# Expert tiles: the second layer in two halves with the next tile's transposes between them, activation copies ahead of weight splits, the last tile in its own PSUM bank

## The reference, cut to what matters

```
attention (decayed linear attention, B=4, H=8, S=768, D=64)  -> x [3072, 512]
x = softplus(x @ w_in [512, 2048]) @ w_out [2048, 512]        dense layer
logits = x @ w_gate [512, 8];  expert_idx = argmax(logits);  gate_w = its softmax value
for e in range(8):                                            routed layer
    xe  = x[expert_idx == e]
    out[expert_idx == e] = gate_w * (relu(xe @ w1[e] [512, 1024]) @ w2[e] [1024, 512])
```

## Time and profile before

| | |
|---|---|
| median of three executions | 1017.44 us |
| the profiled execution | 1015.7 us, its span 1013.9 us |
| TensorE matmuls busy | 985.8 us (97% of the span) |
| VectorE / ScalarE / GpSimd busy | 494.6 / 436.2 / 155.8 us |
| second layer, L1470, 696 matmuls | 167.1 us busy, 6.7 us idle before them |
| first layer, L1445, 696 matmuls | 172.1 us busy, 0.0 us idle before them |
| share of the chain that ended last | PE 89%, DVE 4%, "issue" 3% |

### The profile page before, as it was taken

One profiled execution on the slowest core, in us unless ns is written; L12 is line 12 of the kernel. 1 busy time (PEld: TensorE's weight loads), 2 busy tenths in 40 slices (PEclk: granted clock), 3 DMA queues, 4 the chain that ended last, 5 costly groups with the idle time before them and its releaser, 6 DMA issues.

```text
span 1013.9 us, 17631 instructions
## 1 busy us (share of the span) xinstructions
PE 985.8 (97%) x5968; PEld 854.2 (84%) x5969; DVE 494.6 (49%) x1003; ACT 436.2 (43%) x756; POOL 155.8 (15%) x171
## 2 busy tenths in 40 slices
PE   6999999999999999999999999999999999999995
PEld 5888888888888888888888988888888888888873
DVE  3654464454455455455456696563223423335553
ACT  2764444444444444543544556233223323335541
POOL 3012101001002002001000002022122222233330
PEclk9999999999999999999999999999999999999997
DMA  8523211211111112112111014165111211452830
GB/s 329 188 100 129 74 40 45 65 33 62 59 38 61 45 35 78 42 38 79 30 44 43 32 47 148 48 220 194 50 44 36 112 60 43 187 210 64 334 129 11
DMA packets 28774, 91.83 MB, mean 91 GB/s; under 512 B 4062, under 2 KB 4190, under 8 KB 23584
## 3 DMA queue, kind: packets, MB, share of 16 engines
q1 hardware_dynamic: 23904, 76.48, 21.4%
q0 software_dynamic: 4800, 14.42, 4.4%
HBM read 78.30 MB, written 13.89 MB: 91 GB/s over the span
## 4 chain that ended last, share of the span: by engine, by line
PE 89%; DVE 4%; issue 3%; ACT 1%; DMA 1%; DVEq 1%; ACTq 0%; POOL 0%; SPq 0%; POOLq 0%
PE ps L1356 25%; PE ps L1339 25%; PE ps L1470 15%; PE ps L1445 14%; PE ps L1252 3%; PE ps L1260 2%; PE ps L1455 2%; PE ps L1277 1%; PE ps L1429 1%; PE ps L1269 1%; DVE arena L858 1%; DMA arena<-table 1%; DMA arena<-x_rows,arena 1%; ACT W L692 0%; DVEq L1189 0%
## 5 line engine op out<-in xcount | busy, mean ns | idle before, releaser
L1356 PE MATMUL ps<-W,GS 128*128 128x512 f32 x1152 | 280.0, 396 | 1.8 <-DVE GS L847 1.8
L1339 PE MATMUL ps<-XS,W 128*128 128x384 f32 x1536 | 278.9, 336 | 2.1 <-DVE XS L810 1.6
L1339 PEld LDWEIGHTS ps<-XS,W 128*128 128x128 f32 x1536 | 269.4, 188 | 8.0 <-DVE XS L810 1.8
L1356 PEld LDWEIGHTS ps<-W,GS 128*128 128x128 f32 x1152 | 212.3, 188 | 51.1 <-issue 3.1
L1470 PE MATMUL ps<-W,XS 128*128 (+1 forms) x696 | 167.1, 396 | 6.7 <-DVE XS L1083 6.7
L1445 PE MATMUL ps<-W,XS 128*128 (+1 forms) x696 | 172.1, 396 | 0.0
L843 DVE SCALAR_TENSOR_TENSOR arena<-ps,arena 128x384 f32<-128x384 f32 x128 | 71.3, 557 | 204.7 <-ACT arena L642 204.5
L1470 PEld LDWEIGHTS ps<-W,XS 128*128 128x128 f32 x696 | 129.6, 190 | 34.1 <-issue 8.4
L638 ACT ACTIVATE arena<-ps 128x384 f32<-128x384 f32 x128 | 62.8, 491 | 221.4 <-PE ps L1339 188.8
L1445 PEld LDWEIGHTS ps<-W,XS 128*128 128x128 f32 x696 | 129.6, 190 | 25.8
L858 DVE CUSTOM_DVE_ANT_0 arena<-arena 128x512 bf16<-128x512 f32 x168 | 117.4, 738 | 0.0
(11 more groups left out here) (167 smaller groups left out, 611.0 us busy)
## 6 DMA issues: line engine op xcount, KB each, us to landing
arena<-w SPq DMA_DIRECT2D x32, 1024.0 KB, 6.8
arena<-kT SPq DMA_DIRECT2D x24, 256.0 KB, 2.7
arena<-qT SPq DMA_DIRECT2D x24, 256.0 KB, 3.2
arena<-v SPq DMA_DIRECT2D x24, 256.0 KB, 4.1
arena<-k SPq DMA_DIRECT2D x24, 256.0 KB, 4.3
x_rows<-arena SPq DMA_DIRECT2D x24, 256.0 KB, 4.7
arena<-w_out SPq DMA_DIRECT2D x4, 1024.0 KB, 5.1
arena<-w_in SPq DMA_DIRECT2D x3, 1024.0 KB, 5.1
```

What stands on the lines that cost most here:

```text
L1339: last = pe.matmul(ps_h[g % 2], w_in_s[a][:, g // 4, k_, (g % 4) * P:(g % 4 + 1) * P], xs[half][b][:, k_, :], start=(k_ == 0 and a + b == ...
L1356: last = pe.matmul(ps_x[s], GS[:, g % 2, a, s * P:(s + 1) * P], w_out_s[b][:, g, :], start=(g == 0 and a + b == 0), stop=(g == GF - 1 and ...
```

## The change

- TensorE's tile j becomes: second half of `mm2(j-1)`, `mm1(j+1, 0)`, `mm1(j+1, 1)`, first half of `mm2(j)`, `h_transpose(j+1)`, `x_transpose(j+2)`. `mm2` takes the half n as an argument and counts `s_m2` twice a tile.
- ScalarE's tile j becomes: two `relu(j+1)`, `h_high(j+1, 0)`, `tile_x_high(j+2)`, `h_high(j+1, 1)`, then `refill(j+1, 0)` and `refill(j, 1)`. VectorE's becomes `h_low(j+1, 0)`, `tile_x_low(j+2)`, `scale_y(j)`, `h_low(j+1, 1)`, `refill(j+1, 0)`, `refill(j, 1)`. w2 is thus refilled one iteration after w1 of the same visit, where it was two.
- The slot is computed as `visit & 1` in registers instead of read from a table.
- The last tile's second layer goes to bank 6 and does not wait for bank 5.
- Tiles 4 to 22 are written out on TensorE (no loop). The other engines keep their loops.
- The wait for the last scatter moves from GpSimd to SP.

```diff
@@ -243,7 +243,7 @@
 
         ps_h1 = [ps[:, 3, :], ps[:, 4, :]]
         ps_th = [ps[:, 1, :], ps[:, 2, :]]
-        ps_tx, ps_y2 = ps[:, 0, :], ps[:, 5, :]
+        ps_tx, ps_y2, ps_y_last = ps[:, 0, :], ps[:, 5, :], ps[:, 6, :]
 
         ps_rank0, ps_inv0 = ps[:, 2, 0:(EC + 1) * E], ps[:, 1, 0:5 * TA]
         ps_xT = [ps[:, 5 + i, :] for i in range(SUB)]
@@ -465,6 +465,7 @@
                 load_weights(r, 0)
                 load_weights(r - 1, 1)
             load_weights(E - 1, 1)
+            sp.wait_ge(s_end, 16)
 
 
         @block.gpsimd
@@ -578,7 +579,6 @@
                                     ).then_inc(s_end, 16)
             for q in range(2):
                 pool.wait_ge(s_sc[q], n_sc[q])
-            pool.wait_ge(s_end, 16)
 
 
         @block.scalar
@@ -703,12 +703,11 @@
                     act.wait_ge(s_th, 2 * t)
                 act.activation(h_sb[:, n * 512:(n + 1) * 512], ps_h1[n], ACT.Relu).then_inc(s_relu, 1)
 
-            def h_high(t):
-                for n in range(2):
-                    act.wait_ge(s_th, 2 * t + n + 1)
-                    if not (isinstance(t, int) and t == 0):
-                        act.wait_ge(s_m2, t)
-                    act.activation(th[0][:, n * 512:(n + 1) * 512], ps_th[n], ACT.Copy).then_inc(s_thi, 1)
+            def h_high(t, n):
+                act.wait_ge(s_th, 2 * t + n + 1)
+                if not (isinstance(t, int) and t == 0):
+                    act.wait_ge(s_m2, 2 * t + n - 1)
+                act.activation(th[0][:, n * 512:(n + 1) * 512], ps_th[n], ACT.Copy).then_inc(s_thi, 1)
 
             tile_x_high(0)
             copy_out(NBLK - 1)
@@ -720,13 +719,16 @@
             relu(0, 1)
             tile_x_high(1)
             exp_of(late_wide[0], 2)
-            h_high(0)
+            h_high(0, 0)
+            h_high(0, 1)
             relu(1, 0)
             relu(1, 1)
             tile_x_high(2)
             act.wait_ge(s_sel, 1)
             act.activation(slots.rearrange("p (c w t) -> p c w t", w=2, t=TT)[:, :, 0, :],
                            sel.rearrange("p (c t) -> p c t", t=TT), ACT.Copy, scale=tok).then_inc(s_sl, 1)
+            h_high(1, 0)
+            h_high(1, 1)
 
             def steer(j):
 
@@ -736,25 +738,24 @@
 
                 with act.If(flag > 0):
                     visit = act.value_load(visit_i[0:1, at1(j)], min_val=0, max_val=E - 1)
-                    par = act.value_load(parity_i[0:1, at1(j)], min_val=0, max_val=1)
                     if which:
-                        act.wait_ge(s_m2, j + 1)
+                        act.wait_ge(s_m2, 2 * j + 2)
                     else:
                         act.wait_ge(s_m1, 2 * j + 2)
-                    split_high(visit + 2, bass.ds(par, 1), which)
+                    split_high(visit + 2, bass.ds(visit & 1, 1), which)
 
             def tile(j, ahead=2, refills=True):
-                if refills and ahead >= 1:
-                    before, after = steer(j - 1), steer(j + 1)
-                h_high(j)
-                if ahead >= 1:
-                    relu(j + 1, 0)
-                    relu(j + 1, 1)
+                if refills:
+                    here, after = steer(j), steer(j + 1)
+                relu(j + 1, 0)
+                relu(j + 1, 1)
+                h_high(j + 1, 0)
                 if ahead >= 2:
                     tile_x_high(j + 2)
-                if refills and ahead >= 1:
-                    refill(j - 1, 1, before)
+                h_high(j + 1, 1)
+                if refills:
                     refill(j + 1, 0, after)
+                    refill(j, 1, here)
 
             for j in range(1, TA):
                 tile(j, refills=False)
@@ -765,7 +766,6 @@
             with act.Fori(TA, NT0 - 1) as j:
                 tile(j)
             n_tiles = act.value_load(ntile_i[0:1, 0:1], min_val=NT0, max_val=NT)
-            final = act.value_load(ntile_i[0:1, 1:2], min_val=NT0 - 1, max_val=NT - 1)
             def ending(j):
 
                 with act.If(n_tiles > j):
@@ -775,7 +775,6 @@
                         act.sem_inc(s_left, 1)
 
             ending(NT0)
-            h_high(final)
 
 
         @block.vector
@@ -1076,15 +1075,14 @@
                 dve.wait_ge(s_uhi, t + 1)
                 dve.tensor_tensor(tx[1], ps_tx, tx[0].bitcast(F32), ALU.subtract).then_inc(s_ulo, 1)
 
-            def h_low(t):
-                for n in range(2):
-                    dve.wait_ge(s_thi, 2 * t + n + 1)
-                    cols = slice(n * 512, (n + 1) * 512)
-                    dve.tensor_tensor(th[1][:, cols], ps_th[n], th[0][:, cols].bitcast(F32),
-                                      ALU.subtract).then_inc(s_tlo, 1)
+            def h_low(t, n):
+                dve.wait_ge(s_thi, 2 * t + n + 1)
+                cols = slice(n * 512, (n + 1) * 512)
+                dve.tensor_tensor(th[1][:, cols], ps_th[n], th[0][:, cols].bitcast(F32),
+                                  ALU.subtract).then_inc(s_tlo, 1)
 
             def scale_y(t, q, sc):
-                dve.wait_ge(s_m2, t + 1)
+                dve.wait_ge(s_m2, 2 * t + 2)
                 if sc is not None:
                     dve.wait_ge(s_sc[q], sc)
                 dve.tensor_scalar(y_sb[q], ps_y2, gate_s[:, at1(t)], None, ALU.mult).then_inc(s_y, 1)
@@ -1167,22 +1165,27 @@
             dve.wait_ge(s_lg, 1)
             done(dve.tensor_copy(logits[:, NCH - SUB:NCH, :], by(ps_lg, E)))
             choose(EC, NCH, late, late_wide)
-            h_low(0)
+            h_low(0, 0)
+            h_low(0, 1)
             gate_parts(EC, NCH, late[2], late_wide[0], 2)
             route_tiles()
             tile_x_low(2)
+            h_low(1, 0)
             scale_y(0, 0, None)
+            h_low(1, 1)
             late_indices()
-            h_low(1)
             steering()
+            h_low(2, 0)
             tile_x_low(3)
             scale_y(1, 1, None)
+            h_low(2, 1)
             slot_gates()
-            h_low(2)
+            late_gates()
+            h_low(3, 0)
             tile_x_low(4)
-            late_gates()
+            scale_y(2, 0, 16)
+            h_low(3, 1)
             split_low(1, 1, 0)
-            scale_y(2, 0, 16)
 
             def steer(j):
 
@@ -1191,28 +1194,25 @@
             def refill(j, which, flag):
                 with dve.If(flag > 0):
                     visit = dve.value_load(visit_i[0:1, at1(j)], min_val=0, max_val=E - 1)
-                    par = dve.value_load(parity_i[0:1, at1(j)], min_val=0, max_val=1)
-                    split_low(visit + 2, bass.ds(par, 1), which)
+                    split_low(visit + 2, bass.ds(visit & 1, 1), which)
 
             def tile(j, q, sc, ahead=2):
-                if ahead >= 1:
-                    before, after = steer(j - 1), steer(j + 1)
-                h_low(j)
+                here, after = steer(j), steer(j + 1)
+                h_low(j + 1, 0)
                 if ahead >= 2:
                     tile_x_low(j + 2)
-                if ahead >= 1:
-                    refill(j - 1, 1, before)
                 scale_y(j, q, sc)
-                if ahead >= 1:
-                    refill(j + 1, 0, after)
-
-            h_low(TA - 1)
+                h_low(j + 1, 1)
+                refill(j + 1, 0, after)
+                refill(j, 1, here)
+
+            h_low(TA, 0)
             tile_x_low(TA + 1)
+            scale_y(TA - 1, 1, 16)
+            h_low(TA, 1)
             split_low(1, 1, 1)
             dve.wait_ge(s_tabs, 1)
-            flag = steer(TA)
-            scale_y(TA - 1, 1, 16)
-            refill(TA, 0, flag)
+            refill(TA, 0, steer(TA))
             with dve.Fori(TA // 2, NT0 // 2 - 1) as i:
                 tile(2 * i, 0, 16 * i)
                 tile(2 * i + 1, 1, 16 * i)
@@ -1228,9 +1228,8 @@
                         dve.sem_inc(s_left, 1)
 
             ending(NT0)
-            h_low(final)
-            dve.wait_ge(s_m2, final + 1)
-            dve.tensor_scalar(y_last, ps_y2, gate_s[:, at1(final)], None, ALU.mult).then_inc(s_y, 1)
+            dve.wait_ge(s_m2, 2 * final + 2)
+            dve.tensor_scalar(y_last, ps_y_last, gate_s[:, at1(final)], None, ALU.mult).then_inc(s_y, 1)
 
 
         @block.tensor
@@ -1446,28 +1445,28 @@
                                          start=(k_ == 0 and a + b == 0), stop=(k_ == KD - 1 and a == 1))
                 last.then_inc(s_m1, 1)
 
-            def h_transpose(t, last=False):
+            def h_transpose(t):
                 for n in range(2):
                     pe.wait_ge(s_relu, 2 * t + n + 1)
                     if not (isinstance(t, int) and t == 0):
-                        pe.wait_ge(s_tlo, 2 * t if last else 2 * t + n - 1)
+                        pe.wait_ge(s_tlo, 2 * t + n - 1)
                     for k_ in range(4):
                         last = pe.transpose(ps_th[n][:, k_ * P:(k_ + 1) * P],
                                             h_sb[:, (4 * n + k_) * P:(4 * n + k_ + 1) * P], eye)
```

(77 more changed lines are left out.)

## The result

The changed kernel is slower. Six executions have a median of 1023.87 us (1021.72 to 1031.42) where the kernel before has 1015.91 in the same comparison; the ratio of the means is 1.0094, with a 95% interval of 1.0054 to 1.0135. A second measurement of the same kernel gave 1.0096 (1.0062 to 1.0131, median 1027.34). The forecast was 7.1 us faster.

What follows compares the result with a forecast made beforehand. TensorE's chain of 12.24 us a tile was taken as the bound, winnable only where TensorE stood still; 5.5 + 4.6 - 4.4 + 1.4 = 7.1 us less than the median 1017.4 gives 1010.3, range 1005.0 to 1016.0.

Steps and rivals of the forecast that it cites:

- Part 1: TensorE's second layer waiting for VectorE's low part of h: transposes between the halves remove all 5.5 us of stalls.
- The slack of 1.0 us of the x part: Tightest step of the new order: x part usable at 14.0 us after a tile's start, due for `mm1` at 15.0.
- Part 3: ScalarE's split of late w2 delays `relu` and h transposes in tiles 17, 20, 23, 24: costs 4.4 us, bounds 2.2 and 8.2.
- I take 12.5, between the two, and 10.7 for the third: Assumed us from a burst's first issue on SP to landing of its fourth load (12.5) and third load (10.7).
- the bound of 13.6: Latest landing of a burst's loads, 13.6 us after first issue, when traffic falls off; gives 1.9 us for tiles 17 and 20.
- Part 2: Last tile on TensorE: the 3.5 us lost and 1.4 of low clock go, less 0.28 of issue, a gain of 4.6 us.
- part 4: TensorE's tiles written out, slot from the visit number: extra sequencer work covered by the engine's queue, 0 us.
- (c): Rival outside the forecast's range, counted with anything else that makes the kernel slower; chance 0.08.
- Part 5: End of kernel, last scatter's wait on SP: GpSimd's drain begins right after the issue, the end comes 1.4 us sooner.
- (a): Rival: w2 is never late, 11.5 us less, 1005.9; chance 0.25.
- (b): Rival: the stalls are moved, all bounds against the change and no drain gain, 1.9 us less, 1015.5; chance 0.20.
- The signs to look for: Trace signs, among them w2 splits waiting for DMA in tiles 17 and 20, over 2 us idle around tile 24.

Runs made afterwards that it cites:

- the first experiment: Changed kernel with one edit in SP's queue, w2 of visit r-1 loaded ahead of w1 of visit r: 1009.88 us, ratio to before 0.9937.

## Why the prediction was wrong, point by point

**Part 1, the stalls of VectorE's low part: right.** All 5.5 us went, and a tile without a refill is 12.23 us as computed. The slack of 1.0 us of the x part held: no first layer of the changed kernel waits for it, and with the loads in the new order one does, by 0.42 us, behind the four split pieces.

**Part 3, the late w2: right mechanism, mis-sized, and this decides.** The place, the chain and the tiles were as forecast, as the idle times and the first experiment show. The step that failed is "I take 12.5, between the two, and 10.7 for the third": from the first issue ScalarE could go on after 15.5 and 13.2 us in the first burst, 17.2 and 14.2 in the second. The first issue came at 861.48, 8.69 us after the tile's start at 852.79, where 8.7 was forecast; it is the landing alone. Put into the forecast's own chain, 15.5 and 17.2 give waits of 4.0 and 5.7 us; 3.4 and 5.2 were measured from end to start.

Two readings misled. The largest time to landing, 7.7, does not fit the last load of a burst: issued 3.8 us after the first, it would have landed at 11.5, and the traffic lasted to 13.6. In the changed kernel's profile the same row gives 13.3. And the bound of 13.6 was one burst's; in the burst that begins at 858.47 in the same trace the queues are still full (430 GB/s) at 872. The spacing was short as well: the third and fourth load were issued 0.5 us apart and landed 2.3 and 3.0 us apart, where 1.8 had been taken. The stalls of tiles 17 and 20 became 3.3 and 5.0 us, not 0.1 to 1.9; the one of tile 24 became 3.4, where 2.4 was forecast for tiles 23 and 24 together, and 0 to 1 more for tile 24's own w2.

**A term was missing: the price of the clock behind a new stall.** The prediction charged 1.4 us of it to the old kernel's last tile and nothing to the stalls it forecast itself, which at 1.0 us each would hardly have cost any: behind 1.74 us of idle time in the kernel before, 24 matmuls took 5.75 us, where 5.71 is usual. At 3 to 5 us they cost 8.2 us more between tiles 10 and 27. With 12.9 idle instead of 4.4, and these 8.2, the term is 21.2 where 4.4 stood. That is the slowest of the six executions; how the 7.5 us that separate it from the median divide into idle time and clock, no trace shows. The Trainium skill, "TensorE: Matmul & The Clock Gate", section on oscillation in real kernels, has this as its pattern: idle gaps that let the clock fall, so that the work after each is paid at the low rate. The trace agrees: 4.43 us for twelve matmuls, in a stretch at a mean clock of 0.60, behind a gap of 3.27 us.

**Part 2, the last tile: the copies' cover was right, the gain did not come.** The 2.76 us wait for VectorE is gone and 3.13 us of issue are in its place, with the low clock behind it as before. The step that failed is in part 4, "it has half of its time free" and the 0 that is drawn from it: it looked at addresses and register loads and not at the branch of the ending, 3.5 us in the trace of before, which had 4.2 us of work over it. The change left 2.8 us there, and the branch itself came out at 4.6 us. Its sentence that "the trace shows no such stall here" is true of the loop alone; at the ending the same trace has a branch of 3.5 us that only the engine's queue hid. Why the branch is 4.5 to 4.6 us long in four profiles and 3.3 to 3.9 in the nine others stays open.

**Part 4 otherwise: nearly right.** Written out, tiles 5 to 15 run at 12.23 us each. Rival (c), code fetched behind a burst, is not seen: during the bursts from 861.48 and 904.29 TensorE has no idle time until it waits for ScalarE. The register loads before the ending were not free, they cost the 0.52 us before tile 22's second half.

**Part 5: right size, in part by luck**, 1.6 us against 1.4. The forecast had a drain of 4.97 us begin after the issue. It begins with the issue, 1 us sooner, and takes 1 us more.

**Rivals.** (a) fell with the landing. (b), the stalls moved, was the right kind of answer with bounds too narrow: it had them cost 8.2 us at most. The outcome, slower and not by (c)'s mechanism, had been given a part of 0.08. The signs to look for had named the place, "transposes of h that wait for ScalarE about 1 us", but the line between faster and slower ran through a landing time for which one burst's trace had been taken as a bound.

## What to carry to other kernels

Where a change brings a consumer closer to the load that feeds it, take the time from the first issue of the whole burst to the release of its last load, from every burst in the trace, and put the spread in the range; then look at the order in the queue, for it may remove the question. Price a new TensorE stall with the clock behind it, as a range: in these runs from about 2.6 us on it cost between nothing and 3 us. And when the order of work on an engine changes, list the long instructions of its sequencer (branches above all) with what covers each, and leave a long piece of work in front of them.

## What the runs showed of the hardware that had not been expected

- A branch over the written-out tiles that are not needed took TensorE's sequencer 3.3 to 4.6 us, one that falls through 0.075. TensorE's next matmul started 1.0 to 1.4 us after its end in all thirteen profiles. With 4.2 us of work left at its start 0.28 to 0.40 us of idle time followed, with 3.6 to 3.8 us 0.7 to 1.3 (and in two kernels a second part of 0.8 to 1.0 after four matmuls), with 2.8 us 2.3 to 3.1.
- After idle times of 2.6 to 3.1 us the clock fell in some executions and not in others. It fell after 2.63 (7.37 us for 24 matmuls), 2.76, 2.93, 3.03 and 3.13 (clock 0.83, 0.73 and 0.85 over the next 36), 3.04 and 3.12; it stayed full after 2.75 (5.75 us for 24), 2.86 and 3.06 (8.45 us for 36). After 3.27 to 6.03 it fell each time. After single stalls of up to 2.27 it stayed, but after 1.06 and 0.81 us with four matmuls between them it fell too.
- GpSimd's drain at the end takes 5.0 us if it begins 2.5 us after the last scatter's issue, and 6.0 us if it begins with it.
